# Attention into two MLPs: local scores and minima of the next head pair moved ahead within a step

## What is computed

```python
out_d = sm_attn(q_d, k_d, v_d)                # q, k, v averaged over 4 positions
mask = np.abs(pos[:, None] - pos[None, :]) < 4
scores = np.where(mask, scale * q @ k.T, -1e9)
attn = exp(scores - max) / (sum + 1e-9)
x = np.repeat(out_d, 4, axis=2) + attn @ v
h = (x @ w1) * (x @ w2) @ w3                  # [2304, 512] -> 1024
x = h @ w_out
h = x @ w_in; out = (h * sigmoid(h)) @ w_out2 # 512 -> 2048 -> 512
```

## Time and profile before

| | us |
|---|---|
| median of 3 runs | 823.64 (823.26 to 824.52) |
| the profiled execution, its own time | 822.68 |
| its span | 820.9 |
| attention part, to the first MLP matmul | 156.4 |
| PE busy | 792.4 (97%) |
| DVE busy | 594.2 (72%) |
| ACT busy | 348.4 (42%) |
| POOL busy | 278.6 (34%) |

### The profile page before, as it was taken

The page is one execution under the profiler, slowest core; times in us unless marked ns, Lnnn a source line. Parts: engine busy times, 40 slices in busy tenths (PEclk is TensorE's granted clock), DMA queues, the critical chain, the costliest instruction groups (busy, mean ns, idle before and its releaser), DMA issues.

```text
span 820.9 us, 13901 instructions
## 1 busy us (share of the span) xinstructions
PE 792.4 (97%) x5393; PEld 713.4 (87%) x5393; DVE 594.2 (72%) x949; ACT 348.4 (42%) x791; POOL 278.6 (34%) x342
## 2 busy tenths in 40 slices
PE   7699898999999999999999999999999999999998
PEld 6577677889999899999999889888889988888986
DVE  5787887687676776876769677679777769757644
ACT  6778777533352332443246323344422344432321
POOL 7678887342313333133313123113113212211100
PEclk9799999999999999999999999999999999999999
DMA  8476653111111011101103122122312112412102
GB/s 303 148 231 196 203 172 89 48 69 31 48 52 53 30 48 52 47 32 52 51 26 130 51 87 69 52 78 85 121 63 92 52 52 77 155 52 81 49 0 78
DMA packets 23041, 69.84 MB, mean 85 GB/s; under 512 B 2496, under 2 KB 2496, under 8 KB 22976
## 3 DMA queue, kind: packets, MB, share of 16 engines
q1 hardware_dynamic: 22832, 68.36, 25.5%
q10 hardware_dynamic: 144, 0.59, 0.2%
HBM read 64.23 MB, written 4.72 MB: 84 GB/s over the span
## 4 chain that ended last, share of the span: by engine, by line
PE 83%; POOL 5%; DVE 5%; ACT 4%; issue 2%; DMA 1%; DVEq 0%; POOLq 0%; ACTq 0%
PE ps L1034 43%; PE ps L1092 24%; PE ps L1063 12%; POOL prob_d L413 2%; ACT prob L494 1%; PE ps L1117 1%; DVE low L757 1%; DVE prob L749 1%; POOL vt L383 1%; POOL vd L388 1%; DVE x L793 1%; POOL prob L407 1%; PE ps L1192 1%; DMA qk<-in_qk 1%; ACT prob_d L483 1%
## 5 line engine op out<-in xcount | busy, mean ns | idle before, releaser
L1034 PE MATMUL ps<-xb,wa 128*128 128x384 f32 x2016 | 405.2, 338 | 0.6 <-DVE mu L862 0.5
L1034 PEld LDWEIGHTS ps<-xb,wa 128*128 128x128 f32 x2016 | 355.0, 188 | 22.9 <-DVE mu L862 1.5
L367 POOL TENSOR_TENSOR rw<-rw 128x256 f32<-128x256 f32 x192 | 168.2, 895 | 449.4 <-DMA rw<-in_sets 337.5
L862 DVE TENSOR_TENSOR mu<-ps,mu 128x384 f32<-128x384 f32 x132 | 73.2, 555 | 120.6 <-PE ps L1034 120.3
L1063 PE MATMUL ps<-g,r 128*128 128x512 f32 (+1 forms) x576 | 124.9, 338 | 1.6 <-issue 1.6
L601 ACT ACTIVATE a<-a 128x384 f32<-128x384 f32 x72 | 37.9, 526 | 189.5 <-DVE a L862 189.5
L1092 PE MATMUL ps<-w2h_even,g 128*128 128x512 f32 x432 | 113.2, 394 | 0.0
L1092 PE MATMUL ps<-w2h_odd,g 128*128 128x512 f32 x432 | 112.5, 393 | 0.0
L707 DVE TENSOR_TENSOR wa<-rw,wa 128x1024 fp32r<-128x1024 f32 x96 | 106.4, 1108 | 4.8 <-ACT wa L430 4.6
L1063 PEld LDWEIGHTS ps<-g,r 128*128 128x128 f32 x576 | 97.7, 188 | 10.1 <-issue 2.2
L1092 PEld LDWEIGHTS ps<-w2h_odd,g 128*128 128x128 f32 x432 | 79.9, 188 | 11.9
(11 more groups left out here) (78 smaller groups left out, 745.7 us busy)
## 6 DMA issues: line engine op xcount, KB each, us to landing
rw<-in_sets SPq DMA_DIRECT2D x48, 512.0 KB, 3.5
w2r<-in_w_out SPq DMA_DIRECT2D x24, 512.0 KB, 3.5
qk<-in_qk SPq DMA_DIRECT2D x15, 576.0 KB, 4.8
vg<-in_vg SPq DMA_DIRECT2D x16, 336.0 KB, 5.7
vw<-in_vw SPq DMA_DIRECT2D x16, 320.0 KB, 3.1
out<-osb SPq DMA_DIRECT2D x18, 256.0 KB, 2.5
wn<-in_w SPq DMA_DIRECT2D x16, 256.0 KB, 5.4
raw<-in_w_out SPq DMA_DIRECT2D x2, 1024.0 KB, 9.4
```

Source lines behind the costliest of these rows:

```text
L367: nc.gpsimd.tensor_tensor(blocks[:, o, :], blocks[:, a, :], blocks[:, b, :], op).then_inc(done, 1)
L862: nc.vector.tensor_tensor(o, half_bank(k, i), term, ALU.add).then_inc(sum_ready, 1)
L1034: e = nc.tensor.matmul(ps[:, (k + i) % 2, 0:TH], wa[:, k % 2, l, A_SLOT[i], a * P:(a + 1) * P], xb[:, i, r, a, :], start=(i in (0, 1, 4) a ...
```

## The change

Nothing is computed differently; the steps' contents and order change on all engines.

- TensorE: `scores_local(0)` stands ahead of step 0; step s now holds `scores_local(s+1)`, between the last two parts of `multiply` and `weighted_down`. Both turns stand side by side after two parts of `multiply`. `warm` has fewer transposes in step 2 (14 for 18), and 14 in step 3 where there were none.
- VectorE: `mask_local(s+1)` and `min_local(s+1)` come near the end of step s, and `totals_down(s)` ahead of them in the same step (before: `totals_down(s-1)`, behind the minima of s). `w3_low` comes behind `totals_local`.
- ScalarE: a step begins with `exps_local` and `exps_late`; `copy_pt`, `exps_down`, `copy_ptd`, `take_w3o`, `take_down` follow.
- GpSimd: `shift_local(s+1)` goes behind the down normalisation.
- SyncE: `qk` of pair t+3 is loaded in iteration t, ahead of `vw`.

```diff
@@ SyncE
-                if t + 2 < PAIRS:
-                    load_qk(t + 2)
+                if t == 1:
+                    load_qk(3)
...
+                if t > 0 and t + 3 < PAIRS:
+                    load_qk(t + 3)
@@ GpSimd, step
-                if s + 1 < PAIRS:
-                    shift_local(s + 1)
+                if s == 0:
+                    shift_local(1)
                 pool.wait_ge(inv_d, s + 1)
...
+                if 0 < s < PAIRS - 1:
+                    shift_local(s + 1)
@@ ScalarE, step
+                exps_local()
+                exps_late()
                 for q in splits_of(s):
                     w3_high(q)
...
                 if s > 0:
                     copy_pt()
-                if s > 2:
-                    exps_local()
...
+                exps_down()
                 if s > 0:
                     copy_ptd()
...
+                if s in HIGHS:
+                    first_weights_high(HIGHS.index(s))
                 if s > 0:
                     take_down()
@@ VectorE, step
                     take_local(s - 2)
-                    mask_local(s)
-                    min_local(s)
-                    totals_down(s - 1)
...
-                for q in splits_of(s):
-                    w3_low(q)
                 totals_local(s)
                 if s == 0:
                     min_local(1)
-                    totals_down(0)
...
+                for q in splits_of(s):
+                    w3_low(q)
+                totals_down(s)
...
+                if 0 < s < PAIRS - 1:
+                    mask_local(s + 1)
+                    min_local(s + 1)
+                for q in halves_of(s):
+                    if q % 2 == 1:
+                        take_w3o(q // 2)
@@ TensorE, step
-                scores_local()
-                warm({1: 30, 2: 6}.get(s, 0))
+                warm(FILL[s][0] if s in FILL else 0)
                 scores_down()
-                if s > 0:
-                    turn_local()
-                    warm({1: 4, 2: 6}.get(s, 0))
-                for part in range(3):
+                for part in range(2):
                     for q in qs:
                         multiply(q, part)
                 if s > 0:
+                    turn_local()
+                    warm(FILL[s][1] if s in FILL else 0)
                     turn_down()
-                    warm({1: 5, 2: 6}.get(s, 0))
-                for q in qs:
-                    multiply(q, 3)
+                    warm(FILL[s][2] if s in FILL else 0)
+                for part in range(2, 4):
+                    for q in qs:
+                        multiply(q, part)
+                if s + 1 < PAIRS:
+                    scores_local(s + 1)
                 if s > 0:
                     weighted_down()
                     weighted_local()
```

More of the change, by code:

```diff
@@ L210, in attention_then_mlps @@
         HIGHS = (7, 9)
+        FILL = {1: (30, 4, 2), 2: (6, 6, 2), 3: (6, 6, 2)}
         EXTRA = {8: ("weights", 0), 10: ("tokens", 0), 11: ("weights", 1), 12: ("tokens", 1), 13: ("tokens", 2),
@@ L303, in _ @@
             load_vw(0)
+            load_qk(2)
             for t in range(PAIRS):
[L305 to L306 removed]
+                if t == 1:
+                    load_qk(3)
                 if t + 1 < PAIRS:
@@ L524, in step @@
                     w3_high(HALVES - 3)
+                    copy_pt()
+                    copy_ptd()
                     act.wait_ge(scored, 2 * PAIRS)
@@ L527, in step @@
                     tokens_high(0, 0)
-                    copy_pt()
-                    copy_ptd()
+                    w3_high(HALVES - 2)
                     tokens_high(0, 1)
-                    w3_high(HALVES - 2)
                     act.wait_ge(vt_ready, PAIRS)
                     tokens_high(0, 2)
+                    take_down()
                     take_w3o(MT - 2)
                     w3_high(HALVES - 1)
-                    take_down()
                     act.wait_ge(w3_lo, HALVES)
@@ L843, in _ @@
             take_local(PAIRS - 2)
-            totals_down(PAIRS - 1)
             w3_low(HALVES - 3)
             tokens_low(0, 0)
+            w3_low(HALVES - 2)
             tokens_low(0, 1)
-            w3_low(HALVES - 2)
+            take_local(PAIRS - 1)
             take_w3o(MT - 2)
             w3_low(HALVES - 1)
-            take_local(PAIRS - 1)
             for n in range(3, 7):
@@ L1125, in warm, with scores_local @@
                     nc.tensor.transpose(ps[:, pW, 0:P], ident[:, :], ident[:, :])
+            def scores_local(s):
+                pe.wait_ge(qk_here[s % 3], 16 * (s // 3) + 16)
+                after(pe, masked, s)
+                for g in range(NG):
+                    for h in range(2):
+                        rows = slice(h * D, (h + 1) * D)
+                        for b in range(2):
+                            j = 2 * g + b
+                            e = nc.tensor.matmul(ps[b * BW:(b + 1) * BW, pS + h, g * BW:(g + 1) * BW],
+                                                 qk_at(s)[rows, 0, QS[j]:QS[j] + BW],
+                                                 qk_at(s)[rows, 1, KS[j]:KS[j] + BW],
+                                                 start=True, stop=True)
+                e.then_inc(scored, 1)
             def step(s):
@@ L1138, in scores_down @@
                                                  start=True, stop=True)
[L1139 to L1152, removed]
                     e.then_inc(scored, 1)
@@ L1201, in step @@
                     turn_local()
+                    turn_down()
                     for part in range(2, 4):
                         multiply(qs[0], part)
-                    turn_down()
-                    for part in range(4):
+                    for part in range(2):
                         multiply(qs[1], part)
@@ L1208, in step @@
                     weighted_local()
+                    for part in range(2, 4):
+                        multiply(qs[1], part)
                     for q in qs[2:]:
@@ L1232, in _ @@
             warm(8)
+            scores_local(0)
             for s in range(PAIRS + 1):
```

19 lines of the change are left out of this document (3 added, 16 removed).

## The result

| | before | after |
|---|---|---|
| median, us | 823.87 (823.26 to 824.52, 4 runs) | 818.54 (817.95 to 819.28, 4 runs) |
| the profiled execution, its own time | 822.68 | 818.61 |
| its span | 820.9 | 816.8 |
| first matmul of the MLP part | 156.41 | 151.84 |

The ratio is 0.9936, with a 95% interval of 0.9918 to 0.9953: 5.3 us faster, 3.9 to 6.8. The forecast was 820.8, 2.8 to 3 us faster. In the profiles the attention part ends 4.57 us earlier; the MLP part takes 664.5 us of the span before and 665.0 after, so nothing is won there.

A forecast was written before the change was run, and what follows sets the result against it. A two-step loop of waits, 16.78 us, was taken to bound the attention part. Steps summed to E(15) at 136.6, 5.1 us earlier; after the end, the MLP part starts 2.8 earlier: 820.8 us (819 to 823; full range 816.5 to 826.5).

The forecast's parts named there:

- two-step loop of 16.8 us: Attention part: waits from `turn_local` over ScalarE, mask, minima and GpSimd back to `turn_local`, 16.78 us; the change removes it.
- The rival that the bound stays: Some missed wait keeps a two-step loop of 16.8 us, the end still pays 2.4: 826 us; chance 0.10.
- Loop A: One-step loop over TensorE, from E through `copy_ptd`, `weighted_down`, `weighted_local` and `turn_local` to the next E: 7.6 us.
- The hold: VectorE's `totals_down` is held to the end of GpSimd's normalisation: 0.7 us in a step of 7.6 us.
- E: End of `exps_down` on ScalarE in an attention step; steps run from one to the next, E(15) forecast at 136.6.
- d: Time from E to the end of `totals_down`: 0.3 us undisturbed, 1.0 in a step of 7.6 us.
- loop B: One-step loop over VectorE and ScalarE, from E to the next E: 7.1 us plus any extra plus d.
- The extras: Additional VectorE work in some steps, on loop B: 0.95 us or 1.1 each, 0.7 per low half of `w_out`.
- The end: After E(15), 5.1 us earlier, a part is given back; the MLP part starts at 153.6, 2.8 us earlier.
- More hold: `w3_low` or the extra is held too, 0.8 us later in each of 12 steps: 825 to 829; chance 0.13.
- The clock: TensorE idles before `weighted_down` of step 3 and drops to half clock: 3.5 us for one step, 824.4; chance 0.15.
- The case of no hold: `totals_down` slips ahead of the normalisation or is not held, d stays 0.3: 3.6 us less, 817.2; chance 0.20.

The follow-up runs named there:

- the `w3_low` experiment: The changed kernel with `w3_low` moved behind mask and minima of the next pair: 819.48 us, ratio 0.9953 to the kernel before.

## Why the prediction was right, and what was off

**The bound.** The two-step loop of 16.8 us was there and was broken: the alternation is gone, and so is GpSimd's part in the chain. The masks put back do not bring that loop back; they make another, of one step, at the 10.7 us that the walk gives. The rival that the bound stays did not come.

**Loop A, 7.6, measured 7.8.** One term: `weighted_local` to the next start was taken as 1.09 from the earlier trace rows, where `scores_local` follows. Its line there counts 37 matmuls of 40. The last two of the other three start among the first of `scores_local`, behind its 115.09:

```profile
115.15 0.22 PE L1192 MATMUL ps<-pt,vw 64*64 64x61 f32 x2
```

In the new order `scores_down` follows, all 40 are ahead of it, and it is 1.31 (63.66 - 62.35). All the others are within 0.05: 0.46 to `weighted_down`, 0.93, 0.65, 1.49, 0.53, 0.65, 1.78.

**The hold, 0.7, measured 0.2 in plain steps.** The mechanism was right, the size was not. The normalisation's end came where it was expected, 8.16 us behind the last E (69.12 - 60.96) against 8.3, but E itself came at 7.8 and not 7.6, so that only 0.36 separate them. The term d, from E to the start of what follows `totals_down`, was then 0.5 instead of 1.0 in steps 7, 9 and 11, 0.65 instead of 1.0 in 13 and 15, and 0.4 and 0.3 for 0.35 in 12 and 14. Three small errors took the 0.5 off: 0.2 in E, 0.14 in the normalisation's end, and 0.15 because only the reciprocal follows that end and not the whole ordinary 0.3. That is most of why the steps behind an extra are 8.4 to 8.6 instead of 9.0 to 9.2; another 0.2 a step at most lies in the other terms of loop B. The sign given for the hold, `totd` rows of 0.8 us or more, came in step 1 alone (1.23); they are 0.71 to 0.78 in steps 0, 2 and 3, and 0.17 to 0.50 from step 4 on. Here the walk went wrong in a way that a sum of lengths cannot show: a hold is a difference of two arrival times, and it changes by the whole of each one's error.

**The extras.** They lie on loop B, as forecast, and cost 0.4 to 0.8 a step over A. Step 9 without the extra on the way is 7.81.

**Step 4, 8.8, measured 9.3.** There `totd` was held too (0.78), since GpSimd's normalisation of step 3 began at 35.14; I had put a hold in front of step 3 (d of 0.9) and none behind it. Loop A with the low clock in it was 0.15 later still.

**The end.** Given back was 2.2, forecast 2.3 by the sum (2.4 where the last rival names it); E(15) to the MLP part 16.97 against 17.0. Two errors cancel in it: both `weighted` took 2.70 and not 2.5, the work behind them 14.27 and not 14.5.

**The sum.** E(15) 134.9 against 136.6 is 1.7 of the difference, and MLP starts at 151.84 against 153.6. Behind the 1.7 stand larger errors that partly cancel: steps 4, 5, 6, 8 and 10 are 1.2 us longer than forecast, steps 7, 9 and 11 to 15 are 2.8 shorter. That the time came out within 2.3 us of the forecast is in part luck. The profiled execution's own time fell by 4.07 (forecast 2.8), the medians by 5.3; the difference is that the profiled execution of the kernel before lay 1.19 under its median and that of the changed kernel 0.07 above.

**The rivals.** More hold came in three steps only: `w3_low` took 0.98 and 0.99 us for its 0.63 in steps 5, 9 and 11, behind GpSimd's weight sum, off the longest chain. The clock fell between 36 and 40 us and was 0.91 over 30 to 50. In the changed kernel that cost 0.15 us, since loop B is long there, but the sum assumed the full clock on the path, and the profile of the `w3_low` experiment shows a cost of 1.5 us in the same step. The case of no hold (817.2) was nearer in size than the forecast, though the hold was there.

**A reading that was wrong.** The prediction says that by the rows the other tensor-scalar, `tot`, isn't held. The trace of the kernel before has it held:

```profile
46.31 1.44 POOL L383 TENSOR_TENSOR vt<-vg 112x384 f32<-112x384 f32 x1
...
47.33 0.46 DVE L774 TENSOR_SCALAR tot<-tot 128x10 f32<-128x10 f32 x1
```

It ends at 47.79, 0.04 behind GpSimd's 47.75. In the changed kernel it is 0.27 at most and off the longest chain; in the run with the extras behind the minima it reaches 0.70.

## What to carry to other kernels

Where no engine is full, look in the chain of waits for the loop and count its steps; work for the next item that needs nothing of the present one is worth moving ahead as far as it shortens that loop, and the gain ends at the next loop or at an engine that is full. The next loop can be walked from the distances between starts before anything is run, to 0.2 us for loop A here and to 0.5 for loop B. Check that the instruction whose start ends such a distance does not begin among the last ones of the group. Price what moves to the end of a phase by itself: what is put behind a wait in every step delays the end once more, here by 2.2 us, of which about 1 us was won back by another order in the last step alone. A term that is the difference of two arrivals deserves a range of its own. And a run that adds work to keep a clock up tests the clock only if the clock then is up.

## What the runs showed of the hardware

- A VectorE tensor-scalar over 4 columns, which lasts 0.17 us, lasted up to 1.23 us (step 1 of the changed kernel) while GpSimd's two-input instruction was under way, and ended within 0.03 us of it (19.84 against 19.81; 69.14 against 69.12; 85.59 against 85.56). None of it was seen in the reciprocal of the local sums (0.21 at 99.38, inside GpSimd's weight sum of 99.20 to 99.95), in the reduction `lowd` (0.74 at 96.73, beside `vt` of 96.74 to 97.77) and in the mask read from PSUM (0.88 at 94.36, inside a normalisation of 93.67 to 95.44).
- It goes the other way too: GpSimd's shift of 0.62 lasted 1.52 behind VectorE's extra of 1.2, and its normalisation of 1.26 lasted 1.58 behind a `w3_low` that began 0.16 earlier.
- From the first of the 40 small matmuls of `weighted_local` to the first of what follows it was 1.09 us where 64x64 ones follow, which begin while three of the 40 are still to start, and 1.31 us where 64x144 ones follow.
- TensorE's clock fell for some microseconds between 30 and 40 us in every version (0.54 before, 0.71 to 0.91 in the others), with 14 more transposes (0.83) as without (0.87). At the low level `weighted_down` took 1.81 us for 1.00 and `weighted_local` 2.39 for 1.38.
